# Block attention and two Strassen-multiplied MLPs in one kernel: attention's order in phase A, the blocks that GpSimd makes, and x's high parts

## The reference

```python
def _attn_ref(q, k, v):                      # (8, 8, 576, 64) each
    q_c = q.reshape(B, H, nc, chunk, D)      # chunks of 64 tokens, k_c and v_c likewise
    scores = scale * np.matmul(q_c, k_c.transpose(0, 1, 2, 4, 3))
    scores = scores - np.max(scores, axis=-1, keepdims=True)
    attn = np.exp(scores)
    attn = attn / (np.sum(attn, axis=-1, keepdims=True) + 1e-09)
    return np.matmul(attn, v_c).reshape(B, H, S, D)

def _moe_ref(x, w_in, w_out, alpha):         # x is 4608 x 512, w_in 512 x 2048, w_out 2048 x 512
    h = x @ w_in
    g = np.maximum(h, 0.0) + alpha * np.minimum(h, 0.0)
    return g @ w_out

def _moe2_ref(x, w_in, w_out):
    h = x @ w_in
    return (h - np.tanh(h)) @ w_out
```

## Time and profile before

| | us |
|---|---|
| median of 3 runs | 1727.49 (1724.39 to 1729.89) |
| the profiled execution | 1728.36 |
| its span | 1726.5 |
| TensorE busy in the span | 1552.8 |
| VectorE busy | 1196.1 |
| ScalarE busy | 726.1 |
| GpSimd busy | 542.6 |

### The profile page before, as it was taken

How to read it: one execution, slowest core, us unless ns; L and a number is a source line. 1 busy time by engine, 2 the same in 40 slices (tenths; PEclk the granted TensorE clock), 3 DMA queues, 4 the chain that set the end, 5 groups by cost and what they waited for, 6 DMA issues and landing times.

```text
span 1726.5 us, 30269 instructions
## 1 busy us (share of the span) xinstructions
PE 1552.8 (90%) x11622; PEld 1514.7 (88%) x11622; DVE 1196.1 (69%) x1555; ACT 726.1 (42%) x1379; POOL 542.6 (31%) x754
## 2 busy tenths in 40 slices
PE   6999889986998889899998906999999999999999
PEld 5999889985987889799988906999999999999999
DVE  7998456767865885696796714668668577577575
ACT  5666355354434553553342302324334334235243
POOL 4953437657533323323665582000000000000000
PEclk9999989998998999999999957999999999999999
DMA  6686876895987788778998836776776876867765
GB/s 241 269 293 235 327 251 229 286 317 173 360 295 256 251 314 299 248 267 296 361 310 296 319 109 251 253 293 244 265 292 244 275 274 244 305 246 253 263 251 184
DMA packets 105053, 463.36 MB, mean 268 GB/s; under 512 B 12496, under 2 KB 35024, under 8 KB 62672
## 3 DMA queue, kind: packets, MB, share of 16 engines
q1 hardware_dynamic: 87344, 404.27, 65.6%
q0 software_dynamic: 17280, 56.64, 9.0%
q10 hardware_dynamic: 288, 0.52, 0.1%
HBM read 375.40 MB, written 85.98 MB: 267 GB/s over the span
## 4 chain that ended last, share of the span: by engine, by line
PE 68%; DVE 14%; issue 6%; ACT 6%; DMA 3%; POOL 3%; SPq 0%; DVEq 0%; ACTq 0%; POOLq 0%
PE banks L662 12%; PE banks L663 11%; PE banks L664 11%; PE banks L741 6%; PE banks L743 6%; PE banks L742 6%; DVE go_lo L1281 4%; ACT probs L864 3%; PE banks L734 2%; DVE g_full L1303 2%; PE banks L691 2%; PE banks L735 2%; PE banks L736 2%; PE banks L693 2%; PE banks L692 2%
## 5 line engine op out<-in xcount | busy, mean ns | idle before, releaser
L1281 DVE TENSOR_TENSOR go_lo<-g_full,go_hi 128x768 fp32r<-128x768 f32 x344 | 359.1, 1046 | 205.2 <-ACT go_hi L956 203.2
L662 PE MATMUL banks<-xo_hi,ring 128*128 128x384 f32 x1344 | 462.2, 344 | 6.6 <-DMA ring<-w_split 1.6
L663 PE MATMUL banks<-xo_lo,ring 128*128 128x384 f32 x1344 | 456.1, 339 | 0.0
L664 PE MATMUL banks<-xo_hi,ring 128*128 128x384 f32 x1344 | 455.5, 339 | 0.0
L956 ACT CAST go_hi<-g_full 128x768 fp32r<-128x768 f32 x344 | 284.7, 835 | 311.2 <-PE banks L743 160.5
L741 PE MATMUL banks<-ring,go_hi 128*128 128x256 f32 x1008 | 287.3, 285 | 71.2 <-DMA ring<-w_split 56.5
L742 PE MATMUL banks<-ring,go_hi 128*128 128x256 f32 x1008 | 285.7, 283 | 0.0
L743 PE MATMUL banks<-ring,go_lo 128*128 128x256 f32 x1008 | 285.6, 283 | 0.0
L662 PEld LDWEIGHTS banks<-xo_hi,ring 128*128 128x128 f32 x1344 | 258.3, 192 | 13.0 <-issue 8.5
L741 PEld LDWEIGHTS banks<-ring,go_hi 128*128 128x128 f32 x1008 | 193.8, 192 | 74.1 <-DMA ring<-w_split 56.7
L663 PEld LDWEIGHTS banks<-xo_lo,ring 128*128 128x128 f32 x1344 | 258.1, 192 | 0.0
(11 more groups left out here) (139 smaller groups left out, 2323.0 us busy)
## 6 DMA issues: line engine op xcount, KB each, us to landing
ring<-w_split SPq DMA_DIRECT2D x302, 1024.0 KB, 5.8
w_split<-ring SPq DMA_DIRECT2D x22, 1024.0 KB, 5.4
w_split<-made_first POOLq DMA_DIRECT2D x84, 256.0 KB, 6.2
w_split<-sums POOLq DMA_DIRECT2D x84, 256.0 KB, 5.4
qkv<-in_chunks SPq DMA_DIRECT2D x60, 256.0 KB, 7.2
raw<-in_weights POOLq DMA_DIRECT2D x48, 256.0 KB, 7.2
x_raw<-y_between SPq DMA_DIRECT2D x6, 1536.0 KB, 8.4
out<-stage SPq DMA_DIRECT2D x24, 384.0 KB, 7.1
```

What stands on the lines that cost most here:

```text
L662: nc.tensor.matmul(h, hi, xo_hi[:, o, k, :], start=fresh and k == 0, stop=False, skip_group_check=not fresh)
L663: nc.tensor.matmul(h, hi, xo_lo[:, o, k, :], start=False, stop=False, skip_group_check=not fresh)
L664: last = nc.tensor.matmul(h, lo, xo_hi[:, o, k, :], start=False, stop=k == 1, skip_group_check=not fresh)
L1281: nc.vector.tensor_tensor(go_lo[:, slot, :, :], g_of(s, n), go_hi[:, slot, :, :], ALU.subtract).then_inc(glo_ready, 1)
```

## The change

Five things are done.

1. In phase A of s = 1 to 4 the scores of two units stand after product 5 of an odd pass p = 1, 3, 5, before product 3. Their transposes stand at the head of pass p + 2, ten blocks later, and their outputs after product 1 of that pass. VectorE's and ScalarE's orders follow: the maxima come after `sum_c21`, the first unit is normalized at the end of the pass and the second after `sum_c21` of the next pass, and `activate` and `act_rest` of the pair before are put off by one pass.
2. GpSimd makes its sums in place in the raw weights, in another order, so that both halves of `sums` are free and there are three places for made blocks. Block k waits for the store of block k - 3.
3. `MADE_ORDER` and `pace` change: more blocks in s = 2 to 4 and in phase B of s = 5, fewer in phase A of s = 5 and in s = 6.
4. In phase B of the supers that aren't plain, ScalarE's high parts of x stand at steps 18, 21, 22, 23 and 24 in place of 17, 19, 20, 21 and 23.
5. SP loads q and k of the units of pass 3 one group earlier.

```diff
@@ -164,15 +164,15 @@
 
 
 
-MADE_ORDER = (7, 5, 6, 3, 1, 2, 4)
+MADE_ORDER = (1, 5, 6, 2, 7, 3, 4)
 MADE = [(layer, step_at(step_of(i, p // 2), p % 2) if second else product_at(i, p))
         for layer, second in ((0, True), (1, False), (1, True)) for p in range(PAIRS) for i in MADE_ORDER]
 
 
 def pace(k):
 
-    for s, count, first, tenths in ((1, 14, 2, 37), (1, 28, FIRST_BLOCKS, 10), (2, 16, 2, 30), (2, 8, 60, 60), (3, 14, 2, 37), (3, 6, 60, 80),
-                                    (4, 14, 2, 37), (4, 6, 60, 80), (5, 22, 2, 24), (5, 20, 58, 25), (6, 20, 2, 24)):
+    for s, count, first, tenths in ((1, 14, 2, 37), (1, 25, FIRST_BLOCKS, 12), (2, 19, 2, 26), (2, 8, 60, 60), (3, 16, 2, 32), (3, 8, 60, 60),
+                                    (4, 16, 2, 32), (4, 8, 60, 60), (5, 20, 2, 26), (5, 20, 58, 25), (6, 14, 2, 32)):
         if k < count:
             return s, first + tenths * k // 10
         k -= count
@@ -232,7 +232,7 @@
         sums = sb("sums", [P, 4, 256])
 
         made_first = sb("made_first", [P, 2, 256], F32R)
-        made_second = sums[:, 2:4, :].bitcast(F32R)
+        made_places = (made_first, sums[:, 0:2, :].bitcast(F32R), sums[:, 2:4, :].bitcast(F32R))
         more_sums = made_first[:, :, :].bitcast(F32)
         more_s4 = attnT[:, 0, :, :].rearrange("x b n -> x (b n)").rearrange("x (i n) -> x i n", i=2)
         row_max, row_sum = sb("row_max", [P, 2, 2, G * UNIT]), sb("row_sum", [P, 2, G * UNIT * 2])
@@ -249,7 +249,7 @@
         raw_in = [sem(f"raw_in{i}") for i in range(5)]
         slices_in = [sem(f"slices_in{i}") for i in range(4)]
         raw2_in = [sem(f"raw2_in{i}") for i in range(2)]
-        made_stored = [sem(f"made_stored{i}") for i in range(2)]
+        made_stored = [sem(f"made_stored{i}") for i in range(3)]
         made_step, made_high, made_low = sem("made_step"), sem("made_high"), sem("made_low")
         w_stored = [sem(f"w_stored{i}") for i in range(RING)]
         alpha_in, x_in = sem("alpha_in"), sem("x_in")
@@ -456,6 +456,10 @@
 
             return 0 < s < SUPER - 1
 
+        def late_pair(s, p):
+            first = UPS * (s + 1) + p - 1
+            return (first, first + 1) if phase_a_units(s) and p in (1, 3, 5) else ()
+
         block = ctx.enter_context(nc.Block())
 
         @block.gpsimd
@@ -491,17 +495,17 @@
             def keep_block(k, src):
 
                 layer, j = MADE[k]
-                here = made_second if k % 2 else made_first
+                here = made_places[k % 3]
                 pool.wait_ge(block_done, done(*pace(k)))
-                if k >= 2:
-                    pool.wait_ge(made_stored[k % 2], 16 * (k // 2))
+                if k >= 3:
+                    pool.wait_ge(made_stored[k % 3], 16 * (k // 3))
                 nc.gpsimd.tensor_copy(here[:, 0, :], src).then_inc(made_high, 1)
                 pool.wait_ge(made_high, k + 1)
                 nc.gpsimd.tensor_tensor(here[:, 1, :], src, here[:, 0, :], ALU.subtract).then_inc(made_low, 1)
                 pool.wait_ge(made_low, k + 1)
                 at = j % PER_GROUP * 512
                 nc.gpsimd.dma_start(w_dram[dram_group(layer, j // PER_GROUP, False), :, at:at + 512],
-                                    here.rearrange("x h n -> x (h n)").bitcast(F32)).then_inc(made_stored[k % 2], 16)
+                                    here.rearrange("x h n -> x (h n)").bitcast(F32)).then_inc(made_stored[k % 3], 16)
 
             nc.gpsimd.memset(ident[:], 0.0).then_inc(ident_zero, 1)
             pool.wait_ge(ident_zero, 1)
@@ -527,22 +531,21 @@
                 pool.wait_ge(raw2_in[c % 2], 32 * (c // 2 + 1))
                 quarter = [[raw[:, c % 2, i, m * 256:(m + 1) * 256] for m in range(2)] for i in range(2)]
                 a11, a22 = quarter[0][0], quarter[1][1]
+
                 a12, a21 = (quarter[0][1], quarter[1][0]) if c // PAIRS == 1 else (quarter[1][0], quarter[0][1])
-                s3, s2 = sums[:, 1, :], sums[:, 0, :]
-                nc.gpsimd.tensor_tensor(s3, a11, a21, ALU.subtract).then_inc(made_step, 1)
+                keep_block(k, a11)
+                nc.gpsimd.tensor_tensor(a21, a21, a22, ALU.add).then_inc(made_step, 1)
                 pool.wait_ge(made_step, 4 * c + 1)
-                keep_block(k, s3)
-                nc.gpsimd.tensor_tensor(a21, a21, a22, ALU.add).then_inc(made_step, 1)
+                keep_block(k + 1, a21)
+                nc.gpsimd.tensor_tensor(a11, a21, a11, ALU.subtract).then_inc(made_step, 1)
                 pool.wait_ge(made_step, 4 * c + 2)
-                keep_block(k + 1, a21)
-                nc.gpsimd.tensor_tensor(s2, a21, a11, ALU.subtract).then_inc(made_step, 1)
+                keep_block(k + 2, a11)
+                keep_block(k + 3, a12)
+                nc.gpsimd.tensor_tensor(a21, a22, a11, ALU.subtract).then_inc(made_step, 1)
                 pool.wait_ge(made_step, 4 * c + 3)
-                keep_block(k + 2, s2)
-                pool.wait_ge(made_low, k + 3)
-                nc.gpsimd.tensor_tensor(s2, a12, s2, ALU.subtract).then_inc(made_step, 1)
+                keep_block(k + 4, a21)
+                nc.gpsimd.tensor_tensor(a12, a12, a11, ALU.subtract).then_inc(made_step, 1)
                 pool.wait_ge(made_step, 4 * c + 4)
-                keep_block(k + 3, s2)
-                keep_block(k + 4, a11)
                 keep_block(k + 5, a12)
                 keep_block(k + 6, a22)
 
@@ -753,10 +756,6 @@
                     elif age == 7:
                         output(UPS * (s + 1) + u)
 
-            def late_units(s, p):
-                first = UPS * (s + 1) + p - p % 2 - 2
-                return (first, first + 1) if phase_a_units(s) and p >= 2 else ()
-
             def phase_a(s):
                 product(s, 1, 0)
                 product(s, 1, 1)
@@ -767,22 +766,22 @@
                 product(s, 6, 1)
                 product(s, 4, 0)
                 product(s, 5, 1)
+                for u in late_pair(s, 1):
+                    scores(u)
                 product(s, 3, 0)
                 product(s, 2, 1)
                 product(s, 7, 1)
                 for p in range(2, PAIRS):
+                    for u in late_pair(s, p - 2):
+                        transpose_attn(u)
                     product(s, 6, p)
-                    for u in late_units(s, p):
-                        if p % 2:
-                            transpose_attn(u)
-                        else:
-                            scores(u)
                     product(s, 1, p)
+                    for u in late_pair(s, p - 2):
+                        output(u)
                     product(s, 4, p - 1)
                     product(s, 5, p)
-                    if p % 2:
-                        for u in late_units(s, p):
-                            output(u)
+                    for u in late_pair(s, p):
+                        scores(u)
                     product(s, 3, p - 1)
                     product(s, 2, p)
                     product(s, 7, p)
@@ -1002,34 +1001,31 @@
                     elif age == 7:
                         copy_x(UPS * (s + 1) + u)
 
-            def late_units(s, p):
-
-                first = UPS * (s + 1) + p - p % 2 - 2
-                return (first, first + 1) if phase_a_units(s) and p >= 2 else ()
-
             def phase_a(s):
                 high_parts(s, AHEAD)
                 if s:
                     copy_s1(s, 0)
                     copy_s1(s, 1)
                 for p in range(1, PAIRS):
-                    if p % 2:
-                        for u in late_units(s, p):
-                            place_attnT(u)
+                    for u in late_pair(s, p - 2):
+                        place_attnT(u)
                     if p > 1:
                         high_parts(s, base(p) - 1 + AHEAD)
                         copy_s1(s, p)
+                    if late_pair(s, p - 1):
+                        act_rest(s, p - 2)
                     act_c11(s, p - 1)
-                    for u in late_units(s, p):
-                        if p % 2:
-                            copy_x(u)
-                        else:
-                            exponent(u)
+                    for u in late_pair(s, p - 2):
+                        copy_x(u)
                     if p == PAIRS - 1:
                         high_g(s, 0)
                         high_g(s, 1)
                     high_parts(s, base(p) + 3 + AHEAD)
-                    act_rest(s, p - 1)
+                    if late_pair(s, p):
+                        for u in late_pair(s, p):
+                            exponent(u)
+                    else:
+                        act_rest(s, p - 1)
                     high_parts(s, base(p) + 5 + AHEAD)
                 act_c11(s, PAIRS - 1)
 
@@ -1076,11 +1072,9 @@
                     if s < RUNS - 1:
                         if n in (11, 13):
                             high_x(s + 1, B11 if n == 11 else B21)
-                        elif n == 17:
```

(45 more changed lines are left out.)

## The result

The changed kernel takes 1569.56 us in the median of 4 runs (1568.46 to 1570.40), against 1728.69 us before: the ratio is 0.9079, with a 95% interval of 0.9054 to 0.9104. The forecast was 1570. The profiled execution took 1570.4 us.

What follows compares the result with a forecast made beforehand. TensorE's work was the bound, its idle and half-clock time what could be won: 63 + 58 + 15 - 4 + 13.5 + 14 = 159.5, 2 held back, so 1728 - 158 = 1570 us; range 1548 to 1604.

Steps and rivals of the forecast that it cites:

- Part 1: Phases A of s=1 to 4: attention transposes ten blocks after scores end idle; gain 63 us (bounds 45 and 71).
- the hole of s=2: Phase B of s=2: ring hole closes, 78.6 us to the 63.3 of s=3, gain 15.
- the cost of more making: More blocks made: loss 4 us, of it 3 in s=5 B, 0.5 in s=1 B, 0.5 in s=3 and 4.
- part 3: Phases B, x's high parts at later steps: gain 13.5 us in s=6 to 10 and 14 in s=2 to 5.
- Part 2: Three places and new pace close both ring holes: gain 58 us in s=6 B and 15 in s=2 B.
- landing over places: Making of blocks: with two places landing sets the rate, 4.4 us a block; three would allow 2.9.
- The 2 us held back: Taken off the summed gain for ring loads in denser phases A: 2 us.
- The signs: Changed profile: probs waits under 8 us, clock at least 0.98, phases A 71 to 75, no ring wait over 3.
- the port-bound one: GpSimd without pause holds VectorE: 5 us more in s=5 B, 3 in s=1 B, 1578 us; chance 0.05.

Runs made afterwards that it cites:

- two places: Changed kernel with two places for made blocks in place of three: 1599.8 us, ratio 0.9265.
- the old pace: Changed kernel with the pace table of before, three places and new order of making kept: 1581.35 us, ratio 0.9164.
- both together: Changed kernel with two places for made blocks and the pace table of before: 1614.61 us, ratio 0.9351.
- attention alone: Kernel before with only the change's attention order: 1681.52 us, ratio 0.9758.
- the first of the other pace tables: Changed kernel with a pace table of 20 makes in each phase A of s=1 to 5 and fewer in phase B of s=5: 1559.85 us, ratio 0.904.
- the two runs that take computation and stores apart: Changed kernel, 20 blocks of s=5 B stored without cast or subtraction: 1557.12 us; and with computation, stores, both added in s=7, 8, 9 B: 1588.83 us.
- the makes alone: Kernel before with only the change's makes (sums in place, order of making, three places, pace): 1660.61 us, ratio 0.9633.

## Why the prediction was right, point by point

The span fell by 157.9 us, from 1726.5 to 1568.6; the sum had 159.5 less 2. Its terms, as they stand in the windows:

- **The whole.** That the time came out within 1 us of 1570 is luck. Part 1 was put 5 us too high, the hole of s=2 some 3 (17.3 less the 5.5 of x's high parts is 11.8, against 15), the cost of more making 4 too low, and part 3 10 too low; these cancel. The mechanisms are what holds.
- **Part 1** was 63 and is 57.8 (354.9 to 297.1). The steps hold: idle gone, clock back at 1.00, the chain 9.7 us under ten blocks. s=3 and s=4 are at the 72.9 forecast; the excess is in s=1 and s=2, at 75.8 and 74.9. The waits that I took at 0.7 us a pair come to less in the waits view (4.0 for attnT, 1.4 for u, so 0.45 a pair). Where the missing 5 us went is open. The four phases take 292.7 to 294.7 us, near the forecast 292, in the four traces with this attention order and 60 to 64 blocks made in them (two places, the old pace, both together, attention alone), and 297.1 with the 68 of the changed kernel. A cost of denser making there, which the sum has at nothing, would fit. But the first of the other pace tables has 80 blocks in them and takes 297.2 all the same, so it is not shown.
- **Part 2**, s=6 B, was 58 and, with the share of x's high parts in it taken off, is 61.7 - 3.6 = 58.1. s=2 B fell by 17.3 (15 and 3.5 forecast). The mechanism, landing over places, is shown by the two places, where GpSimd's waits for stores are back, and the pace table's share by the old pace; the two together agree. Mis-sized was GpSimd's rate: 3.48 us a block from k=114 to 161 (3.2, 3.6 and 2.9 forecast by stage), so k=161 landed 174.6 us after s=5 began, not 163. SP asked for it after 183.2, not 177, as s=5 B and s=6 A were longer too, and so it was 8.6 us early, not 14. In s=2 the block came 1.1 us late, not 6 early: 22 blocks in the 74.9 us of s=2 A are 3.4 us each, not 2.9. GpSimd's busy time there is now 58.67 / 22 = 2.7 us a block where I took 2.4, and the rest are the gaps that I had and 6.9 us of waits for stores. A ring load's spare time covered the 1.1 us.
- **What more making costs**: 4 was forecast. s=1 B rose by 1.8, s=5 B came out at 69.4, so 3.5 for x's high parts and 3 for the makes nearly cancel as forecast. But both were too small there: undoing the high parts costs 6.6, and the makes alone cost 7.
- **Part 3** was 27.5 and is the worst-sized term: undone it costs 37.7. In s=7 the gain is 3.6 us and not 2.7, since the whole idle went and some 0.6 more; in the first layer it is 3.9 to 6.6.
- **The 2 us held back**: phases A of s=5 and s=6 grew by 0.9 and 1.1 us. That is the size forecast, but in the two runs that take computation and stores apart, where s=5 A and s=6 A have the same work, s=5 A is 60.4 in both and s=6 A 60.9 and 60.7, so it may be chance. TensorE waited 3.3 us in all for ring loads, three times.
- **The signs.** In the phases A no transpose waits, the clock is 1.00, and three of the four lengths are within 71 to 75 us (s=1 A is 75.8). No ring wait is over 1.6 us. A made block costs 61.2 / 17 = 3.6 us in s=5 A and 69.4 / 19 = 3.7 in s=5 B (2.9 to 3.6 forecast). One thing did happen that I had named as being wrong, a ring load in s=1 to 6 that lands after 12 us. In s=1 to s=6 A of the changed kernel:

```profile
DMA to landing us min/median/max: 4.7/7.9/13.6
```

The sign was badly chosen. The earlier trace rows has only the loads of s=5 and s=6 A; over the same stages as here the kernel before had such loads too:

```profile
DMA to landing us min/median/max: 4.7/7.4/15.6
```

What a late load costs is what TensorE waits for it, and that stayed small.

Of the rivals, the port-bound one was the one to keep. VectorE has next to no idle time in s=5 B, and its go_lo is held more than before (in two views, with the mean in ns behind the busy time in the second):

```profile
L1275 DVE TENSOR_TENSOR go_lo<-g_full,go_hi x26: 946/1489/1720, 780.7 to 844.6; 128x768 fp32r<-128x768 f32 x26
...
L1275 DVE TENSOR_TENSOR go_lo<-g_full,go_hi 128x768 fp32r<-128x768 f32 x26 | 35.3, 1361 | 0.0
```

The mean went from 1.236 us to 1.361, which is 0.40 us over the undisturbed 0.958: just the delay that this rival had. Its price for the makes in s=5 B held as well, 3 + 5 = 8 us against the 7 measured, but not in s=1 B, 0.5 + 3 = 3.5 against 1.8. It did not show in the total because part 3 brought 10 us more than forecast.

GpSimd is held as well. Its subtraction of 256 columns, in s=5 A and in s=5 B:

```profile
L504 POOL TENSOR_TENSOR sums<-raw,sums x12: 729/737/1402, 724.0 to 779.0; 128x256 fp32r<-128x256 f32 x12
...
L504 POOL TENSOR_TENSOR sums<-raw,sums x13: 1322/1328/1347, 779.0 to 846.7; 128x256 fp32r<-128x256 f32 x13
```

It takes 0.74 us in the median in s=5 A, where VectorE is busy for 41.9 of 61.2 us, half of it with sums that read a bank in PSUM, and 1.33 in s=5 B, where VectorE hardly rests and mostly makes go_lo and g_sum, which read SBUF alone. I had set the rule of the Trainium skill, "SBUF — State Buffer", section "SBUF: two separate sides", against a mean of 1.236 us and called it far from doubling. That reading was wrong: GpSimd's operation is the shorter one, so a go_lo held for one whole subtraction is longer by 0.74 us and not doubled, and 0.958 + 0.74 = 1.70 is close to the longest, 1.72. The trace agrees with the lock that the page describes, and I gave it too little. Stores without computation do not bring it on (0.958 us); beside computation they add to it (1.348 against 1.147).

In the hole of before, 256 KB stores landed in 2.7 us. The Trainium skill, "DMA: Bandwidth & Descriptors", section "Anatomy of one DMA — SWDGE (gpsimd) path", gives 2.0 us and the bytes over 436 KB a microsecond, so an estimate of 2.6 us: the trace agrees for that hole, in which TensorE waits and no ring load is under way. Beside the ring's traffic in s=5 A it is 6.4, and it is this number that the number of places has to be reckoned with.

Open: the sums in place were not run apart from the third place, for which they free the room; that they cost nothing is argued from the same count of operations. The new order of making and the earlier load of q and k were not run alone either.

## What to carry to other kernels

Reckon a producer's time for a block as the larger of its own work and (work + landing) over its places, with the landing of the loaded stage (for two places 4.4 us was reckoned here, and with two places again a block took 63.0 / 14 = 4.5 us in s=5 B and 60.4 / 12 = 5.0 in s=5 A), and compare blocks owed with time left at each deadline; a part that makes the consumer faster moves those deadlines forward, as attention alone showed. Put GpSimd's elementwise work where VectorE has slack: its computation holds VectorE, and its stores alone did not. And follow a moved instruction one queue further than its first reader: the tightest chain behind the second normalize ran through two engines to attnT.
